# Attention and two FFN layers on one core: where a pair's inverse sums are stored, spread and inverted

## The reference

```python
q_rot, k_rot = rotate(q), rotate(k)            # rotary embedding, 4 x 8 heads, 576 x 64
scores = q_rot @ k_rot.T / sqrt(64)
attn = exp(scores - max(scores)); attn = attn / (sum(attn) + 1e-9)
x = (attn @ v)                                 # to (2304, 512)
h = x @ w_in;  x = (h - tanh(h)) @ w_out       # first FFN, 512 x 2048
h = x @ w_in2; out = (h * sigmoid(h)) @ w_out2 # second FFN, 512 x 2048
```

## Time and profile before

| | us |
|---|---|
| median of 3 runs | 1104.51 |
| profiled execution | 1107.88 |
| its span in the trace | 1106.0 |
| TensorE busy | 1064.7 (96%) |
| VectorE busy | 435.3 (39%) |
| ScalarE busy | 412.1 (37%) |
| GpSimd busy | 282.8 (26%) |

### The profile page before, as it was taken

The page is one execution under the profiler, slowest core; times in us unless marked ns, Lnnn a source line. Parts: engine busy times, 40 slices in busy tenths (PEclk is TensorE's granted clock), DMA queues, the critical chain, the costliest instruction groups (busy, mean ns, idle before and its releaser), DMA issues.

```text
span 1106.0 us, 18105 instructions
## 1 busy us (share of the span) xinstructions
PE 1064.7 (96%) x7404; PEld 997.6 (90%) x7404; DVE 435.3 (39%) x696; ACT 412.1 (37%) x760; POOL 282.8 (26%) x127
## 2 busy tenths in 40 slices
PE   3889999989999999999999999999999999999998
PEld 2879888879999999999999999899989989899897
DVE  5556666656252323232232333523223232322322
ACT  2557776666722323223232322323223232232322
POOL 6667897966470000000000015700000000000000
PEclk9999999999999999999999999999999999999999
DMA  5445455453151000000000004200000000000000
GB/s 194 161 140 157 143 147 179 143 160 84 38 188 52 1 1 0 0 0 0 0 0 0 0 0 152 77 1 28 0 0 28 0 28 0 0 28 0 28 0 29
DMA packets 36368, 60.54 MB, mean 55 GB/s; under 512 B 15712, under 2 KB 18016, under 8 KB 34400
## 3 DMA queue, kind: packets, MB, share of 16 engines
q1 hardware_dynamic: 36320, 59.87, 17.0%
HBM read 50.46 MB, written 4.79 MB: 50 GB/s over the span
## 4 chain that ended last, share of the span: by engine, by line
PE 82%; DMA 8%; SPq 3%; POOL 3%; DVE 2%; ACT 1%; issue 1%; ACTq 0%; POOLq 0%; DVEq 0%
PE ps L722 35%; PE ps L741 18%; PE ps L736 17%; DMA inverse_sums<-rinv 4%; PE ps L592 3%; PE ps L556 2%; PE ps L586 2%; DMA R<-inverse_sums 2%; DMA sums<-ev 1%; PE ps L496 1%; PE ps L622 1%; SPq L282 1%; DVE hm L919 1%; POOL xT L412 1%; PE ps L546 1%
## 5 line engine op out<-in xcount | busy, mean ns | idle before, releaser
L722 PE MATMUL ps<-xs_h,win_l 128*128 128x384 f32 x768 | 258.6, 337 | 1.4 <-DVE xs_l L979 1.4
L722 PE MATMUL ps<-xs_h,win_h 128*128 128x384 f32 x768 | 257.6, 335 | 0.0
L722 PE MATMUL ps<-xs_l,win_h 128*128 128x384 f32 x768 | 257.1, 335 | 0.0
L884 ACT ACTIVATE g_h<-ps 128x384 fp32r<-128x384 f32 x192 | 94.4, 492 | 306.1 <-PE ps L741 135.1
L878 ACT ACTIVATE act<-ps 128x384 f32<-128x384 f32 x192 | 94.5, 492 | 247.7 <-PE ps L722 247.6
L722 PEld LDWEIGHTS ps<-xs_h,win_l 128*128 128x128 f32 x768 | 144.2, 188 | 7.5 <-issue 3.9
L722 PEld LDWEIGHTS ps<-xs_l,win_h 128*128 128x128 f32 x768 | 144.2, 188 | 3.5
L722 PEld LDWEIGHTS ps<-xs_h,win_h 128*128 128x128 f32 x768 | 144.1, 188 | 0.0
L919 DVE TENSOR_REDUCE hm<-ps 128x2 f32<-128x576 f32 x144 | 108.5, 756 | 63.4 <-PE ps L496 56.8
L736 PE MATMUL ps<-g_h,wout_h 128*128 128x384 f32 x384 | 128.3, 334 | 0.0
L736 PE MATMUL ps<-g_h,wout_l 128*128 128x384 f32 x384 | 128.3, 334 | 0.0
(11 more groups left out here) (86 smaller groups left out, 1619.6 us busy)
## 6 DMA issues: line engine op xcount, KB each, us to landing
raw<-qk SPq DMA_DIRECT2D x15, 1152.0 KB, 5.9
w_stage<-w_in SPq DMA_DIRECT2D x8, 1024.0 KB, 5.0
w_stage<-w_out SPq DMA_DIRECT2D x8, 1024.0 KB, 5.2
v<-vfull SPq DMA_DIRECT2D x16, 384.0 KB, 4.1
R<-inverse_sums SPq DMA_DIRECT2D x32, 144.0 KB, 3.1
out<-ostage SPq DMA_DIRECT2D x5, 768.0 KB, 3.5
vr<-vin SPq DMA_DIRECT2D x16, 192.0 KB, 3.2
ev<-ev SPq DMA_DIRECT2D x16, 144.0 KB, 2.3
```

What stands on the lines that cost most here:

```text
L722: last = mm(o, w[g][:, kk, c:c + 128], x[:, kk, :], start=(n == 0), stop=(n == 11))
L884: nc.scalar.activation(g_h[f % 2][:, :], ps[:, 4 + f % 4, 0:TN], ACT.Copy, scale=(1.0, 0.5)[L]).then_inc(s_gh, 1)
```

## The change

SyncE handles gather, join, store and spread of pair n-1 in iteration n; the store comes behind the join, the spread behind the rows of maxima. The last two pairs' extra loop behind the main one is left with pair 15 alone. VectorE takes `invert(n-1)` behind place S7, ahead of the low part of unit 7.

```diff
             for n in range(PAIRS):
                 if n + 3 < PAIRS:
                     load(n + 3)
-                if n >= 2:
-                    store_inverse(n - 2)
                 if n + 1 < PAIRS:
                     load_split_v(n + 1)
-                if n >= 2:
-                    spread_inverse(n - 2)
+                if n >= 1:
+                    gather_sums(n - 1)
                 if 1 <= n < PAIRS - 1:
                     load_full_v(n + 1)
                 if n >= 1:
-                    gather_sums(n - 1)
                     join_heads(n - 1)
+                    store_inverse(n - 1)
                 if n + 1 < PAIRS:
                     max_rows(n + 1)
+                if n >= 1:
+                    spread_inverse(n - 1)
                 if n + 2 < PAIRS:
                     sp.wait_ge(s_lq, n + 3)
                     copy_blocks(n + 2, slice(0, 4), s_bd[n % 2])
                 if n in W_LOAD:
                     load_w(W_LOAD[n])
-            for n in (PAIRS - 2, PAIRS - 1):
-                if n == PAIRS - 1:
-                    gather_sums(n)
-                    join_heads(n)
-                store_inverse(n)
-                spread_inverse(n)
+            n = PAIRS - 1
+            gather_sums(n)
+            join_heads(n)
+            store_inverse(n)
+            spread_inverse(n)
...
                 x_place(n, "S6", "S7")
+                invert(n - 1)
                 low(9 * n + 7)
                 x_place(n, "S8", "A5")
-                invert(n - 1)
```

## The result

| us | before | after |
|---|---|---|
| median of 20 runs | 1103.04 (1097.48 to 1107.02) | 1108.55 (1106.04 to 1111.51) |
| ratio, 95% interval | | 1.0049 (1.0037 to 1.0060) |
| profiled execution, its span | 1107.88, 1106.0 | 1108.64, 1106.7 |

The change costs 5.5 us. The forecast was 4.3 us less. Nearly every mechanism of the forecast stands in the new trace, and yet its sign is wrong; the spans of the two profiled executions differ by only 0.7 us, the medians by 5.5. The gap between those two differences is the first trace of the kernel before, whose execution lay 4.8 us above the median, which took a second and a third trace to see.

A forecast was written before the change was run, and what follows sets the result against it. The store-and-spread ring, not TensorE, was taken to set ordinary attention pairs' period. Period changes of -5.8 us plus 1.5 for the clock gave -4.3: 1107.88 to 1103.6, then 3.4 lower for the median, 1100.2; range 1089 to 1110.

The forecast's parts named there:

- The ring is cut: SyncE stores pair n-1's inverse sums after its gather, landing in 1.4 us, not 4.9; R then reaches GpSimd before normalise.
- both waits of the earlier trace: GpSimd's 56.5 us wait for R and ScalarE's 13.4 us wait for normalise; both should nearly vanish.
- The rows of maxima wait for the reciprocal: On SyncE they stand behind the store, which waits for VectorE's reciprocal: 1.2 us more per pair, ordinary period 15.9 us.
- Weight loads hold v: In pairs 2, 9 and 12 ScalarE waits for split v behind the weight load; period 18.8 us each.
- The clock: Term: 0.5 us for each weight-load pair, 1.5 in all. Rival: pauses swing the clock in ordinary pairs, 1117.4 us (0.06).
- The sum: New minus old periods over pairs 2 to 13, -5.8 us; with 1.5 added for the clock, -4.3 us.
- The copies' cover is thin: Diagonal copies behind the spread land near when TensorE's rest row scores want them; costed 0 to 0.35 us, taken 0.1.
- The last step: From the profiled execution's forecast 1103.6 us to the median 1100.2, as the old one lay 3.4 above its three-run median.
- Heal: Rival: v is not held behind the weights, so pairs 2, 9 and 12 take 15.9 us; 1090.0 us; chance 0.14.
- Free maxima: Rival: the wait for the rows of maxima costs nothing, 1.2 us less in eleven pairs; 1087 or below; chance 0.04.
- Late copies: Rival: a slower store delays spread, diagonal copies and rest row scores 1.2 us in eleven pairs; 1113 us; chance 0.10.

The follow-up runs named there:

- the quick traces: No edit: the kernel before, profiled a second and a third time; 1099.2 us and 1099.98 us.
- The three places of the invert: The changed kernel with VectorE's invert one step earlier (1095.12 us), as changed (1108.55 us) and one step later, behind unit 7's low part (1123.19 us).
- the run with all three moves: The changed kernel with rows of maxima and diagonal copies ahead of the store, and split v ahead of raw and weights; 1087.51 us, ratio 0.9858.
- the fastest kernel: SyncE order split v, raw, gather, full v, weights, maxima, copies, join, store, spread; invert last, as in the kernel before; 1085.18 us, ratio 0.9833.

## Why the prediction was wrong

**The ring is cut.** Right: landing 1.5 us, both waits of the earlier trace rows down or gone. GpSimd's wait was to fall under 15 us and fell to 23.9, which costs nothing. That the store's late landing by itself sets the period of an ordinary pair is not borne out: with a median landing of 1.8 us in place of 4.9, in the kernel before, the five pairs took 75.1 us, no less than in the quick traces, since the ring over the split v is about as long.

**The rows of maxima wait for the reciprocal.** Right in place and size: 3.28 us against 3.3 from the S7 maximum to the first scores, 15.9 us for an undisturbed pair. The three places of the invert (14.8, 15.9 and 16.9 us a pair) show it.

**Weight loads hold v.** Right: 19.5, 19.2 and 18.7 against 18.8, with ScalarE waiting 2.1, 3.4 and 2.3 us for v.

**The clock.** The sum allowed 0.5 us for a drop in each of the three pairs with a load; one fell, pair 9 (0.91).

**The copies' cover is thin: the term that was too small.** The sum took 0.1 us and let the second copy land in 2.2 us, the median, or 2.7 at most. In four pairs it took longer and TensorE's rest row scores waited: 3.0 us ahead of pair 3 (wait 0.33), 3.8 ahead of pair 10 (1.44), 3.2 ahead of pair 12 (0.83) and 3.3 ahead of pair 14 (1.01), which the sum had at 0 because no maxima are left there, though its rest row scores remain. The two copies ahead of pair 10:

```profile
L282 SPq DMA_DIRECT2D hl<-hl x2: 623/642/662, 198.4 to 199.1; - x2
...
DMA to landing us min/median/max: 2.7/3.3/3.8
```

ScalarE's wait for v in pairs 6 and 8 (1.1 and 0.6 us) was not in the sum either, since v was priced for the pairs with a weight load alone. From pair 2 to 15 the sum had 219.75 - 5.8 + 1.5 = 215.5 us; measured 218.84, 3.4 us more: 4.9 us in the periods (1.3 in pairs 10 and 11, 1.2 in pair 14, 1.0 in the pairs with a load, 0.8 in the five, 0.6 in pair 3), less the 1.5 set aside for the clock.

**The old times came from a single trace, well above the median: a second step that failed.** The last step, "It was 3.4 us above the median of the three runs, so the median comes to 1100.2", moved both kernels by the same amount. But those 3.4 us (4.8 against the median of 20) sat in the very periods that the change was credited with shortening: 65.75 us for the three pairs where the quick executions have 58, and 77.4 for the five where they have 75, a good part of the former being half-clock time. The same new periods set against the second and third traces give +5.1 and +3.9 us where the first gave -5.8; a median execution lies between, at about 0 if one reads it off in proportion to the three execution times (an estimate). The profiled execution of the changed kernel (1108.64), by contrast, lies on its median.

**The account.** From the forecast 1100.2 to 1108.55 are 8.4 us, of which 3.4 is this step, 3.4 the periods, and 1.6 small shifts of start, pair 15 and FFN between single executions (1.0 - 0.4 + 1.0). A further 1.5 of the missed difference is the median of before, 1103.04 in 20 runs for 1104.51 in three. Neither error turns the sign by much alone: -4.3 with the 4.8 of the first trace (1107.88 - 1103.04) put right is +0.5, and with the 5.0 of periods and shifts +0.7, which is the difference of the two profiled spans. Together they make the +5.5. That 1108.55 lies within the forecast range of 1089 to 1110 doesn't speak for the sum, whose direction was wrong.

**The rivals.** None came true as priced. Heal: no, shown by the waits for v. Free maxima: no. Late copies: in small part, 3.8 us in all rather than 13, and not by the store, which landed in 1.5 us. The clock: no, it kept 1.00 in ordinary pairs though each has a pause of 0.8 us. The Trainium skill's warning of a swinging clock under frequent micro-idles (TensorE: Matmul & The Clock Gate, the section on a second failure mode) is not borne out here with pauses of 0.8 us every 16, nor with 1.9 us every 17, where the ordinary pairs kept 1.00 too.

What stays open is why the kernel before spreads so widely from one execution to the next; its three traces have ScalarE waiting 13.4, 7.1 and 7.7 us for normalise, though the store's median landing is 4.9 to 5.0 us in all three and the longest 7.7 to 8.2. The clock has a part in it: the first trace has a mean granted clock of 0.991, the quick ones 0.996, and of the 54 other executions whose clock is known the two slowest (1108.38 and 1106.77 us) have 0.991 too, but one of 1101.26 has 0.992. Whether a longer wait brings on the lower clock or the other way round isn't shown. Nor is it why a copy sometimes takes 3 to 4 us to land.

## What to carry to other kernels

On an engine that issues its DMAs in order, a step moved ahead brings its wait with it: ask what stands behind it and at what time that is needed, and place the engine work it waits for first. Here the same SyncE order is 0.5% slower or 0.6% faster by one line on VectorE. A gain counted from waits seen in a single trace needs a second trace, since the waits that vary from run to run are the ones that a lone profile over- or understates; the shift to the median isn't the same for both kernels. And where the cover is thin, a landing is to be priced by its slow cases and not by its median.

## What the runs showed of the hardware beyond that

A 4.5 KB store takes 1.4 us to land on a quiet queue and up to 8.2 behind 2 MB (weights and raw), and in the run with all three moves two 2.2 KB gathers issued behind 2 MB took 7.4 and 8.0 us. The place in the queue decides most of a small transfer's time, but not all: landings are not strictly in the order of issue. In pair 9 of the changed kernel the first gather, issued at 183.72, landed at 189.27, ahead of the raw load issued at 181.21 (190.07) and the split v issued at 181.75 (190.40). In the fastest kernel the queue moved 166 GB/s on average over pairs 3 to 13, with nine of these eleven pairs at 14.7 us.
